# First mixture layer: block products by Strassen's rule in the first product, tokens in thirds outside

## What is computed

```python
def _moe_ref(x, w_gate, w1, w2):          # x is 1536 x 512, w1 8 x 512 x 1024, w2 8 x 1024 x 512
    logits = x @ w_gate
    logits = logits - logits.max()
    P = np.exp(logits)
    for _ in range(8):
        P /= P.sum(1, keepdims=True) + 1e-09
        P /= P.sum(0, keepdims=True) + 1e-09
        P *= N / E
    for e in range(E):
        h = np.maximum(x @ w1[e], 0.0)
        ye = h @ w2[e]
        out += P[:, e:e + 1] * ye
```

## Time and profile before

| what | value |
|---|---|
| median of 3 runs (lowest, highest) | 1465.86 us (1463.57, 1466.82) |
| profiled execution | 1457.44 us |
| its span | 1455.7 us |
| TensorE busy | 1403.6 us, 96% |
| VectorE busy | 530.6 us, 36% |
| ScalarE busy | 346.1 us, 24% |
| GpSimd busy | 173.1 us, 12% |
| mean granted TensorE clock | 0.981 |

### The profile page before, as it was taken

One profiled execution on the slowest core, in us unless ns is written; L12 is line 12 of the kernel. 1 busy time (PEld: TensorE's weight loads), 2 busy tenths in 40 slices (PEclk: granted clock), 3 DMA queues, 4 the chain that ended last, 5 costly groups with the idle time before them and its releaser, 6 DMA issues.

```text
span 1455.7 us, 18813 instructions
## 1 busy us (share of the span) xinstructions
PE 1403.6 (96%) x7522; PEld 1183.9 (81%) x7522; DVE 530.6 (36%) x1435; ACT 346.1 (24%) x667; POOL 173.1 (12%) x168
## 2 busy tenths in 40 slices
PE   7998999999999999999999999999999975999997
PEld 5886888888888888888888888888888854899997
DVE  5555623233232323233232323233232346887000
ACT  5763211211020211202120211211020211444422
POOL 4540201001010101001010101101010100012111
PEclk9999999999999999999999999999999985999999
DMA  8660201010110101010110101010100023665430
GB/s 189 166 169 32 87 1 58 0 58 0 58 53 5 58 0 58 0 58 0 58 58 0 58 0 58 0 58 1 57 0 0 0 87 127 243 235 189 157 129 23
DMA packets 77266, 94.04 MB, mean 65 GB/s; under 512 B 37280, under 2 KB 43424, under 8 KB 77216
## 3 DMA queue, kind: packets, MB, share of 16 engines
q1 hardware_dynamic: 75168, 87.09, 18.4%
q0 software_dynamic: 2048, 6.29, 1.4%
HBM read 87.08 MB, written 6.29 MB: 64 GB/s over the span
## 4 chain that ended last, share of the span: by engine, by line
PE 90%; DVE 3%; ACT 3%; issue 1%; POOL 1%; DMA 1%; SPq 0%; DVEq 0%; POOLq 0%; ACTq 0%
PE PS L1388 24%; PE PS L1387 24%; PE PS L1389 24%; PE PS L1522 6%; PE PS L1505 5%; PE PS L1331 2%; DVE G L1150 1%; PE PS L1552 1%; PE PS L1312 1%; PE PS L1302 1%; ACT sc L629 1%; PE PS L1469 1%; ACT pt L636 0%; PE PS L1480 0%; PE PS L1488 0%
## 5 line engine op out<-in xcount | busy, mean ns | idle before, releaser
L672 ACT ACTIVATE hhi<-PS 128x512 fp32r<-128x512 f32 x192 | 114.8, 598 | 850.9 <-PE PS L1389 850.9
L1388 PE MATMUL PS<-xlo,w1hi 128*128 128x512 f32 x768 | 299.5, 390 | 0.0
L1387 PE MATMUL PS<-xhi,w1hi 128*128 128x512 f32 x768 | 299.5, 390 | 0.0
L1389 PE MATMUL PS<-xhi,w1lo 128*128 128x512 f32 x768 | 299.4, 390 | 0.0
L1389 PE MATMUL PS<-w2hi,hlo 128*128 128x512 f32 x768 | 298.8, 389 | 0.0
L1387 PE MATMUL PS<-w2hi,hhi 128*128 128x512 f32 x768 | 298.8, 389 | 0.0
L1388 PE MATMUL PS<-w2lo,hhi 128*128 128x512 f32 x768 | 298.8, 389 | 0.0
L957 DVE SCALAR_TENSOR_TENSOR hlo<-PS,hhi 128x512 fp32r<-128x512 f32 x192 | 132.7, 691 | 353.1 <-ACT hhi L672 352.9
L973 DVE SCALAR_TENSOR_TENSOR acc<-PS,prob_e,acc 128x512 f32<-128x512 f32 x180 | 135.1, 751 | 333.4 <-PE PS L1389 333.4
L490 POOL TENSOR_TENSOR w2lo<-raw,w2hi 128x512 fp32r<-128x512 f32 x64 | 81.6, 1307 | 903.8 <-ACT w2hi L569 896.7
L1387 PEld LDWEIGHTS PS<-xhi,w1hi 128*128 128x128 f32 x768 | 144.6, 188 | 30.2
(11 more groups left out here) (221 smaller groups left out, 1114.1 us busy)
## 6 DMA issues: line engine op xcount, KB each, us to landing
raw<-in_w SPq DMA_DIRECT2D x34, 1024.0 KB, 6.1
expert_weights<-in_w SPq DMA_DIRECT2D x10, 2048.0 KB, 11.2
raw<-in_w SPq DMA_DIRECT2D x6, 2048.0 KB, 11.1
vs<-in_v SPq DMA_DIRECT2D x16, 192.0 KB, 3.2
x_rows<-acc SPq DMA_DIRECT2D x3, 1024.0 KB, 8.3
vw<-in_v SPq DMA_DIRECT2D x16, 120.0 KB, 3.1
qs<-in_qT SPq DMA_DIRECT2D x4, 384.0 KB, 4.0
kp<-in_kT SPq DMA_DIRECT2D x4, 384.0 KB, 4.7
```

The lines of the kernel that those rows point to most:

```text
L672: act.activation(hhi[:, slot, k, 0:width], PS[:, bank, 0:width], ACT.Relu).then_inc(s_done, 1)
L1387: T.matmul(o, whi, xh, start=first, stop=False)
L1388: T.matmul(o, whi, xl, start=False, stop=False)
L1389: return T.matmul(o, wlo, xh, start=False, stop=last)
```

## The change

The chunk of tokens is now the outside loop, and the experts the inside one, so all weights are loaded and split three times. In `h_products` both operands of a unit are cut into 2 x 2 quarters (the 512 inputs in two, the 512 hidden columns in two, the 512 tokens in two), and the four quarters of the result are made from seven block products instead of eight, of sums and differences of the quarters. Each part is 12 matmuls of 256 columns. The sums of the weights (`w1_sums`, four per unit) are made by VectorE; those of the tokens (`x_sums`, four per chunk) by GpSimd, for the first chunk by VectorE. ScalarE then casts seven parts (`w1_hi`, `x_hi`) and VectorE makes seven low parts (`w1_lo`, `x_lo`). Some partial results serve in two quarters of h: ScalarE copies three of them out of PSUM (`part_copy`), VectorE adds them to others (`h_add`). `y_products` is as before but in banks 3, 4, 5 and 7. The low part of the second weights stays on GpSimd (`w2_lo`), now once per unit, but for the first unit, where VectorE makes it.

In the attention the transposed `x` is now copied plainly (`x_copy`) and nothing is subtracted there. The gate logits are made from this copy in plain float32, 12 matmuls in place of 24. The tokens of `x` and the output `acc` share their room.

```diff
+        def quarters(m, n):
+            return [m[:, 2 * a:2 * a + 2, b * n:(b + 1) * n] for a in range(2) for b in range(2)]
...
+        def x_parts(c):
+            a11, a21, a12, a22 = quarters(xT0[:, c], HC)
+            s1, s3, s2, s4 = (x_sum[:, n] for n in range(SUMS))
+            return [a11, s1, s2, a12, s3, s4, a22]
...
+        def w1_parts(par):
+            b11, _, b21, b22 = quarters(raw1[:, par], FQ)
+            t1, t3, t2, t4 = (w1_sum[:, n] for n in range(SUMS))
+            return [b11, t1, t2, b21, t3, b22, t4]
+        PART_SUM = [0, 1, 3, 0, 2, 0, 4]
+        PART_BANK = [0, 1, 0, 2, 0, 1, 0]
+        PART_OPENS = [True, True, False, True, False, False, False]
+        Y_BANKS = [3, 4, 5, 7]
...
+            def load_w1(e, half, u, first=False):
+                if not first:
+                    sp.wait_ge(s_w1l, of_unit(e, PARTS, u - 1, 0))
+                sp.dma_start(raw1[:, half], w1_v[e, :, :, half * FH:(half + 1) * FH]).then_inc(s_raw1[half], 16)
...
+                with sp.Fori(0 if c else 1, E) as e:
+                    for half in range(2):
+                        load_w1(e, half, c * UNITS + half)
+                        load_w2(e, half, c * UNITS + half)
+                if c:
+                    store_x1(c - 1)
...
-            pool.tensor_copy(w1hi[:, 0], raw1[:, 0]).then_inc(s_hi1, 1)
+            for n in range(PARTS):
+                if PART_SUM[n]:
+                    pool.wait_ge(s_wsum, PART_SUM[n])
+                pool.tensor_copy(w1hi[:, n], w1_parts(0)[n]).then_inc(s_w1h, 1)
...
-            with pool.Fori(0, E) as e:
-                split_lo2(1, e * 2 + 1)
-                split_lo2(0, e * 2 + 2)
+            def w2_lo(i, u):
+                pool.wait_ge(s_w2h, of_unit(i, 1, u, 1))
+                for k in range(FC):
+                    ins = pool.tensor_tensor(w2lo[:, u % 2, k], raw2[:, u % 2, k], w2hi[:, u % 2, k].bitcast(F32), ALU.subtract)
+                ins.then_inc(s_w2l, 1)
+            for c in range(NC):
+                if c + 1 < NC:
+                    x_sums(c + 1)
+                if c == 0:
+                    w2_lo(0, 1)
+                with pool.Fori(0 if c else 1, E) as i:
+                    for half in range(2):
+                        w2_lo(i, c * UNITS + half)
...
+            def part_copy(i, u, n, at, bank):
+                act.wait_ge(s_pd, of_unit(i, PARTS, u, at))
+                act.copy(h_sum[:, n], PS[:, bank, :].rearrange("p (f n) -> p f n", f=2)).then_inc(s_rc, 1)
+            def h_hi(i, u, q):
+                fs, ts = H_QUARTER[q]
+                if q < 3:
+                    act.wait_ge(s_c, of_unit(i, 3, u, q + 1))
+                    h = h_sum[:, q]
+                else:
+                    act.wait_ge(s_pd, of_unit(i, PARTS, u, PARTS))
+                    h = PS[:, 0, :].rearrange("p (f n) -> p f n", f=2)
+                act.activation(hhi[:, u % 2, fs, ts], h, ACT.Relu).then_inc(s_hh, 1)
+            def period(i, u, more, x=None):
+                part_copy(i, u, 0, 1, 0)
+                part_copy(i, u, 1, 2, 1)
+                part_copy(i, u, 2, 3, 0)
+                for q in range(4):
+                    if more and q < 3:
+                        w1_hi(i, u + 1, q)
+                    h_hi(i, u, q)
+                for n in range(3, PARTS):
+                    if more:
+                        w1_hi(i, u + 1, n)
+                if x is not None:
+                    for n in range(PARTS):
+                        x_hi(x, n)
+                w2_hi(i, u)
...
+            x_hi(0, 0)
+            act.wait_ge(s_gg, 1)
+            act.copy(group_rows[:], PS[0:GROUP * NC, GROUPS_BANK[0], :]).then_inc(s_ggc, 1)
+            for n in range(1, PARTS):
+                x_hi(0, n)
...
+            def h_add(i, u, q):
+                at, bank = [(4, 2), (5, 0), (6, 1)][q]
+                dve.wait_ge(s_pd, of_unit(i, PARTS, u, at))
+                dve.wait_ge(s_rc, of_unit(i, 3, u, q + 1))
+                V.tensor_tensor(h_sum[:, q], PS[:, bank, :].rearrange("p (f n) -> p f n", f=2), h_sum[:, q], ALU.add
+                                ).then_inc(s_c, 1)
...
+            def h_period(i, u, more):
+                if more:
+                    for n in range(SUMS):
+                        w1_sums(i, u + 1, n)
+                        yield
+                h_add(i, u, 0)
+                yield
+                if more:
+                    w1_lo(i, u + 1, 0)
+                    yield
+                h_add(i, u, 1)
+                yield
+                h_lo(i, u, 0)
+                yield
+                h_add(i, u, 2)
+                yield
+                for q in range(1, 4):
+                    h_lo(i, u, q)
+                    yield
+            def y_period(i, u, more, x, ys):
+                ys = iter(ys)
+                for n in range(PARTS):
+                    if more and n:
+                        w1_lo(i, u + 1, n)
+                        yield
+                    if x is not None:
+                        x_lo(x, n)
+                        yield
+                    if n in (2, 4, 6):
+                        next(ys, None)
+                        yield
+                if u == 0:
+                    for k in range(FC):
+                        w2_lo(i, u, k)
+                        yield
+                for _ in ys:
+                    yield
...
+            dve.wait_ge(s_oh, XT_DONE + 2)
+            a11, a21, a12, a22 = quarters(xT0[:, 0], HC)
+            s1, s3, s2, s4 = (x_sum[:, n] for n in range(SUMS))
+            V.tensor_tensor(s1, a21, a22, ALU.add).then_inc(s_xsum, 1)
+            V.tensor_tensor(s3, a11, a21, ALU.subtract).then_inc(s_xsum, 1)
+            dve.wait_ge(s_xsum, 1)
+            V.tensor_tensor(s2, s1, a11, ALU.subtract).then_inc(s_xsum, 1)
+            dve.wait_ge(s_xsum, 3)
+            V.tensor_tensor(s4, a12, s2, ALU.subtract).then_inc(s_xsum, 1)
+            aside = first_units()
+            next(aside)
...
-                h_lo(it, 0, it // FC, it % FC, it % 3, CH, s_hh, s_hl)
+                next(aside, None)
...
+            def three(o, whi, wlo, xh, xl, first, last, shared=False):
+                T.matmul(o, whi, xh, start=first, stop=False, skip_group_check=shared)
+                T.matmul(o, whi, xl, start=False, stop=False, skip_group_check=shared)
+                return T.matmul(o, wlo, xh, start=False, stop=last, skip_group_check=shared)
+            def h_products(i, u, x=None):
+                for n in range(PARTS):
+                    pe.wait_ge(s_w1l, of_unit(i, PARTS, u, n + 1))
+                    if x is not None:
+                        pe.wait_ge(s_xl, PARTS * x + n + 1)
+                    if n == 0 and u:
+                        pe.wait_ge(s_hl, of_unit(i, 4, u, 0))
+                    if n == 2:
+                        pe.wait_ge(s_rc, of_unit(i, 3, u, 1))
+                    if n == 4:
+                        pe.wait_ge(s_rc, of_unit(i, 3, u, 3))
+                    if n == 5:
+                        pe.wait_ge(s_rc, of_unit(i, 3, u, 2))
+                    if n == 6:
+                        pe.wait_ge(s_c, of_unit(i, 3, u, 2))
+                    for f in range(2):
+                        fs = slice(f * P, (f + 1) * P)
+                        for k in range(2):
+                            ins = three(PS[:, PART_BANK[n], f * HC:(f + 1) * HC], w1hi[:, n, k, fs], w1lo[:, n, k, fs],
+                                        xhi[:, n, k, :], xlo[:, n, k, :], PART_OPENS[n] and f == 0 and k == 0, k == 1, True)
+                    ins.then_inc(s_pd, 1)
+            def y_products(i, u):
+                pe.wait_ge(s_w2l, of_unit(i, 1, u, 1))
+                pe.wait_ge(s_hl, of_unit(i, 4, u, 4))
+                for k in range(TC):
+                    pe.wait_ge(s_acc, of_unit(i, TC, u, k + 1))
+                    ts = slice(k * P, (k + 1) * P)
+                    for f in range(FC):
+                        ins = three(PS[:, Y_BANKS[k], :], hhi[:, u % 2, f, ts], hlo[:, u % 2, f, ts], w2hi[:, u % 2, f, :],
+                                    w2lo[:, u % 2, f, :], f == 0, f == FC - 1)
+                    ins.then_inc(s_y, 1)
+            def layer1(c, i, last):
+                h_products(i, c * UNITS + 1)
+                y_products(i, c * UNITS)
+                if not last:
+                    h_products(i, c * UNITS + 2)
+                elif c < NC - 1:
...
+                    h_products(i, c * UNITS + 2, c + 1)
+                y_products(i, c * UNITS + 1)
```

More of the change, by code:

```diff
@@ L1420, in _ @@
[L1420 to L1428 removed]
+                pe.wait_ge(s_x1c, (d + 1) * NC)
+                gate_products(1, [d], lambda c, d: x1T[:, d, c * CH:(c + 1) * CH])
             x1_transposes(0)
@@ L1435, in _ @@
             x1_logits(2)
[L1436 to L1441 removed]
+            x1_logits(3)
+            logit_columns(1)
             def prefixes(c, a):
```

478 lines of the change are left out of this document (223 added, 255 removed).

## The result

The changed kernel takes 1454.47 us (median of 4 runs, 1453.47 to 1455.33), the kernel before, run beside it, 1464.87 us (1463.57 to 1466.82). The ratio is 0.9928 with a 95% interval of 0.991 to 0.9945: faster by 0.72%, 10.4 us, where 24 were forecast. The direction is right and the time lies in the range of 1428 to 1464, but outside the likeliest case's own 1435 to 1452. The profiled execution took 1455.33 us.

The account below looks back on a forecast made before the run. TensorE was taken to bound the kernel. From the last copy of x through the middle layer 1031.6 us against 1054.1, 22.5 less, plus 1.5 in the attention: 24.0 off 1465.86, predicted as 1442, range 1428 to 1464.

Parts of the forecast that it names:

- the likeliest case: Whole kernel: pitch 0.1145 us, 24.0 us less, predicted 1442, own range 1435 to 1452; chance 0.62.
- The price of the 256-column matmul: In h_products: 0.1145 us per matmul, bounds 0.1133 and 0.120; unit 20.50 us against 21.76.
- a sign of being wrong: Steady part of the middle layer: a period over 20.9 us, where 20.5 was forecast.
- Rival (1): 256-column matmuls: pitch 0.120 from a fixed cost per matmul, 21.3 us more, 1463, no change; chance 0.10.
- The walk of the start: Middle layer's start: part 7 of unit 2 starts 48.5 us after the last copy of x; TensorE stands 30 us.
- the sign: Start of the middle layer: pauses summing to much other than 23 to 27 us would show the prediction wrong.
- The chunk changes: Middle layer, twice: VectorE makes the next unit's additions late by 6.5 us, then 3.5; 10.0 together.
- Fetches and clock: Middle layer: +2 us for an instruction wait after the attention's branch, +5 for lower-clock matmuls after three pauses.
- The attention: VectorE's nine waits for casts, 19.5 us, go away; 1.5 us booked as gain, bounds 0 and 4.
- The other engines keep up: Steady period of 20.50 us: VectorE needs 18.1 to 19.2, ScalarE 10.3, so TensorE sets the period.
- Rival (2): Hand-overs inside a unit: TensorE stops at parts 3, 5 and 7; at 0.4 us each +56, 1498; chance 0.12.
- Rival (3): 256-column matmuls: pitch of 107 to 111 ns, 29 to 14 us less, 1413 to 1428; chance 0.04.

Follow-up runs that it names:

- the streams: Changed kernel with streams of 64 matmuls of a kind put before the first part; fp32r with 128 weight columns: 227 ns for 512 columns, 120 for 256.
- after_sink1: Changed kernel with one scaling round instead of eight; 1036.8 us from the last copy of x to the end of the last product, against 1050.3.
- before_sink1: Kernel before with one scaling round instead of eight; 1054.9 us from the last copy of x to the end of the last product, against 1054.1.
- before_again: Kernel before, unchanged, profiled once more; span 1461.0 us, last product of the middle layer at 1176.57, 284.5 us behind it.

## Why the prediction was half right

Its sum was -24.0 us; the measured -9.0, up to the last product of the layer. The difference of 15.0 goes over its steps so:

- **The price of the 256-column matmul: +21.3.** This is the step that failed. I took 0.1145 and held 0.120 for the upper bound, with a chance of 0.10; it is 0.120, the period 20.98 and so over the 20.9 that I had named as a sign of being wrong, and 46 x 84 x 0.0055 = 21.3. The argument was that records of 256 columns are 112 ns shorter than those of 512, so the pitch is too. The two records were of unlike matmuls: those of 278 ns have 64 rows and start in pairs. In the streams, where both have 128 rows, 256 columns have 283 ns and 512 have 389, 106 apart, and so are the pitches (227 - 120 = 107); with 64 rows the record is 280 over the same pitch of 120. A length alone gives no pitch either: the 192-column stream has records of 273 ns and a pitch of 111, and 256 bf16 columns have the same 273 and a pitch of 109. The starts in the earlier trace rows were 0.12 apart, to a hundredth, and that was the better row. The sentence that the weight load "just fits" was right and of no use, as it wasn't the pace. Rival (1) had this price right, and 1463; what it lacked were the gains below.
- **The walk of the start: -0.8.** The last part of unit 2 was to start 48.5 us after the last copy; it started at 165.86, 47.75 after it. The places of the pauses and their order came as described, but not their lengths: 6.9 us before the last part of unit 1 (10 forecast), 4.3 before unit 2 (6), 4.4 before its last part (6), 15.7 together where I had named 23 to 27 as the sign. VectorE's walk came out and TensorE's share of it didn't: its products between the pauses took longer than counted, at a granted clock of 0.84 and 0.77. after_sink1 shows the reason given, rounds without cover, and before_sink1 that they had it.
- **The chunk changes: +1.7.** 10.0 forecast; 7.3 + 4.35 = 11.65 measured over a period. Taking `w2_lo` from GpSimd won back 3.5 of them, so the meetings were part of it.
- **Fetches and clock: -3.4.** 7 booked. From 165.86 to 1168.46 it is 1002.6 us; 46 x 10.08 + 1.44 + 48 x 10.88 = 987.4, and the chunk changes take 11.65, which leaves 3.6. After the pauses the clock was at 0.50 from 166 to 170 us, as the earlier trace rows had led to expect; its falls before that, which I had booked on top of the walk, lay inside it.
- **The attention: -3.8.** 5.3 us for the 1.5 booked; I had given bounds of 0 and 4. "TensorE is nearly full there" was too strong a reason for so little: from 20 to 118 us TensorE was idle for 6.2 us before and for 2.4 after. That it was the waits of the earlier trace rows that gave the 5.3 is not shown.

That the time came no further from 1442 is in part luck: the other four steps together were off by 6.3 us the other way, and with the price alone put right the sum gives 1463.

The other engines keep up, as was worked out: VectorE needs 16.3 us of a period (78% of 20.98), less than the 18.1 to 19.2 of the walk. Rival (2), the hand-overs inside a unit, didn't come: TensorE has no gap in the two long stretches. Rival (3), a pitch of 107 to 111, falls with the 120.

## What to carry to other kernels

Cutting products into smaller ones pays the fixed part of every matmul again: seven block products in place of eight should save an eighth of 10.88 us a unit, 1.36, and 48 x 0.2267 - 84 x 0.1200 = 0.80 was left. Take a pitch from the distance of many starts of a like matmul, not from the records of unlike ones, and where the trace has no such stretch, weigh the fixed cost as the likely case. Then look for the places where the old products hid other engines' work: the steady periods kept up without a gap, but the start lost 15.7 us, and moving operations, without leaving any out, made the kernel 6.7 us shorter, at the start and at the chunk changes.

## What the runs showed that I had not expected

- fp32r matmuls cost more than their columns (13 to 14 ns with 128 weight columns and 256 to 512 moving), bf16 ones 2.5; and the extra depends on the weight columns in no simple way (120, 116, 113, 118 for 128, 96, 64, 32).
- A stretch of 280 us with the same instructions takes 277.9 to 285.2, in before_again for the most part by one line of VectorE that was released up to 2.2 us late three times, by what the profile doesn't say.
- Twelve operations that cost 0.3 us as work cost 12 us or more when each first waits for another engine's copy (two of them also took 3 us, beside GpSimd).
